# Diagonal sums of the first five chunks: from a row-wise product on GpSimd and a reduction on VectorE to a channel-wise product and a matmul

## The reference

```python
state = zeros((B, H, D, D))                      # B=2, H=8, S=768, D=48
for t in range(S):
    cur = einsum('bhd,bhe->bhde', u[None] * kt, vt)
    y[:, :, t] = einsum('bhd,bhde->bhe', rt, state + cur)
    state = wt[:, :, :, None] * state + einsum('bhd,bhe->bhde', kt, vt)
```

## Time and profile before

| what | value |
|---|---|
| median of three runs | 377.11 us |
| profiled execution | 376.72 us |
| its span | 375.1 us |
| PE busy | 365.7 us (97%) |
| DVE busy | 166.1 us (44%) |
| ACT busy | 107.7 us (29%) |
| POOL busy | 193.1 us (51%) |
| mean granted TensorE clock | 0.991 of full speed |

### The profile page before, as it was taken

The page is one execution under the profiler, slowest core; times in us unless marked ns, Lnnn a source line. Parts: engine busy times, 40 slices in busy tenths (PEclk is TensorE's granted clock), DMA queues, the critical chain, the costliest instruction groups (busy, mean ns, idle before and its releaser), DMA issues.

```text
span 375.1 us, 6472 instructions
## 1 busy us (share of the span) xinstructions
PE 365.7 (97%) x2546; PEld 325.7 (87%) x2546; DVE 166.1 (44%) x278; ACT 107.7 (29%) x205; POOL 193.1 (51%) x198
## 2 busy tenths in 40 slices
PE   5999899999999999999999999999999999999996
PEld 5888778888799998999999998888888888888885
DVE  6799888754501332295449363350023300133100
ACT  3677345555552006420012123240012200122000
POOL 3799999997967447579999970019000000000000
PEclk9699999999999999999999999999999999999999
DMA  7988696411033000031134400000000000000011
GB/s 233 417 290 328 245 367 244 148 56 44 2 108 103 3 0 3 0 84 44 43 86 126 134 36 2 0 1 31 28 28 2 0 28 30 28 0 2 0 41 45
DMA packets 12033, 31.94 MB, mean 85 GB/s; under 512 B 1633, under 2 KB 4962, under 8 KB 12002
## 3 DMA queue, kind: packets, MB, share of 16 engines
q1 hardware_dynamic: 12000, 31.51, 24.2%
q10 hardware_dynamic: 2, 0.00, 0.0%
HBM read 29.15 MB, written 2.36 MB: 84 GB/s over the span
## 4 chain that ended last, share of the span: by engine, by line
PE 74%; DVE 0%; issue 0%; POOL 0%; DVEq 0%
PE bank L1212 24%; PE bank L1210 24%; PE bank L1211 24%; PE bank L1320 1%; POOL yt L652 0%; DVE x L1055 0%; DVE x2T L1125 0%; DVEq L227 0%; DVEq L1053 0%
## 5 line engine op out<-in xcount | busy, mean ns | idle before, releaser
L854 ACT ACTIVATE ha_hi<-bank 128x512 fp32r<-128x512 f32 x36 | 21.6, 599 | 106.7 <-PE bank L1212 106.7
L1116 DVE SCALAR_TENSOR_TENSOR ha_lo<-bank,ha_hi 128x512 fp32r<-128x512 f32 x36 | 24.9, 692 | 50.6 <-ACT ha_hi L854 50.6
L1210 PE MATMUL bank<-ha_hi,c_lo 128*128 128x512 f32 x108 | 42.1, 390 | 0.0
L1212 PE MATMUL bank<-u2T_hi,c_hi 128*128 128x512 f32 x108 | 42.0, 389 | 0.0
L1211 PE MATMUL bank<-u2T_lo,c_hi 128*128 128x512 f32 x108 | 42.0, 389 | 0.0
L1212 PE MATMUL bank<-ha_hi,c_hi 128*128 128x512 f32 x108 | 42.0, 389 | 0.0
L1210 PE MATMUL bank<-u2T_hi,c_lo 128*128 128x512 f32 x108 | 42.0, 389 | 0.0
L1211 PE MATMUL bank<-ha_lo,c_hi 128*128 128x512 f32 x108 | 42.0, 389 | 0.0
L1211 PE MATMUL bank<-sg_lo,z_hi 128*128 128x384 f32 x96 | 32.1, 334 | 0.0
L1210 PE MATMUL bank<-sg_hi,z_lo 128*128 128x384 f32 x96 | 32.1, 334 | 0.0
L1212 PE MATMUL bank<-sg_hi,z_hi 128*128 128x384 f32 x96 | 32.1, 334 | 0.0
(11 more groups left out here) (143 smaller groups left out, 849.6 us busy)
## 6 DMA issues: line engine op xcount, KB each, us to landing
turned<-in_turned_all SPq DMA_DIRECT2D x10, 772.0 KB, 7.5
rows<-in_rows_all SPq DMA_DIRECT2D x12, 576.0 KB, 5.6
raw<-in_moe_w_ch SPq DMA_DIRECT2D x12, 384.0 KB, 3.1
raw<-in_moe_w_sg SPq DMA_DIRECT2D x6, 384.0 KB, 3.3
out<-x2T SPq DMA_DIRECT2D x8, 256.0 KB, 2.0
raw<-in_moe_w_in SPq DMA_DIRECT2D x4, 384.0 KB, 6.7
raw<-in_moe_w_tok SPq DMA_DIRECT2D x4, 384.0 KB, 3.1
check_w<-in_w SPq DMA_DIRECT2D x2, 576.0 KB, 11.6
```

The source lines that it names most:

```text
L854: sc.activation(ha[0][:, i, :], bank[:, :], ACT.Relu).then_inc(act_out, 1)
L1116: ve.scalar_tensor_tensor(ha[1][:, i, :], bank[:, :], 0.0, ha[0][:, i, :].bitcast(F32), ALU.max, ALU.subtract).then_inc(dve_out, 1)
L1210: te.matmul(dst, left[1], right[0], start=first, stop=False)
L1212: return te.matmul(dst, left[0], right[0], start=False, stop=last)
```

## The change

For chunks 0 to 4 the diagonal sums are made in another way. For the other chunks all stays, with the counts of the semaphores shifted by five.

- GpSimd multiplies r and k by channel (`rk_by_channel`, 112x512, both from `turned`). The product lies in the part of the `rows` slot where k and r by token lay.
- TensorE multiplies that, pair by pair and 64 tokens at a time, with two columns of u (8 matmuls with a moving side of two columns), into bank b2 behind the turned k. They stand in `turn_kp`, before its semaphore.
- ScalarE's `take_k` copies 8 columns more, into `kn_dg`, and from chunk 1 on waits for `diagonal_v` of the chunk before.
- `rk_products`, `rku_products` and `diagonal` no longer run for chunks 0 to 4; chunks 0 to 4 load v alone by token (192 KB in place of 576 KB).
- u by pairs comes with the first w (8 columns more); `ub` is loaded by a broadcast DMA after `load_rows(4)`; `spread_u`, its zeroed row, its DMA and its copy go.
- VectorE runs `forward(1)` before the masks of chunk 0.
- `keep_busy`: 14 at the start in place of 13; the two that stood in each of chunks 1 to 4 go, and two more stand in chunk 0.

```diff
+            def rk_by_channel(n):
+                if n == 0:
+                    pool.wait_ge(k0_in, 16)
+                    pool.wait_ge(r0_in, 16)
+                else:
+                    wait_turned(pool, n)
+                if n >= NR:
+                    pool.wait_ge(kn_turned, states(n - NR))
+                gp.tensor_tensor(rkc(n), kr_tile(n, 1), kr_tile(n, 0), ALU.mult).then_inc(rkc_done, 1)
...
             scale_k(0)
             scale_first_r()
-            rk_products(0)
-            for n in range(YR):
-                if n:
-                    diagonal_v(n - 1)
-                    scale_r(n + 1)
-                    scale_k(n + 1)
-                else:
-                    scale_k(1)
-                    rku_products(0)
-                    scale_r(1)
-                if n == YR - 1:
-                    diagonal_v(n)
-                rk_products(n + 1)
-                rku_products(n + 1)
+            rk_by_channel(0)
+            scale_k(1)
+            scale_r(1)
+            rk_by_channel(1)
+            for n in range(1, YR):
+                diagonal_v(n - 1)
+                if n + 1 < YR:
+                    rk_by_channel(n + 1)
+                scale_r(n + 1)
+                scale_k(n + 1)
+            diagonal_v(YR - 1)
+            rk_products(YR)
+            rku_products(YR)
             scale_k(YR + 1)
...
             def take_k(n):
-                sc.copy(kn[:, :, :], pairs(b2, QP)).then_inc(kn_copied, 1)
+                m = NP * QP
+                if n < YR:
+                    m += H
+                    if n:
+                        act.wait_ge(base_done, n)
+                sc.copy(kn_dg[:, 0:m], b2[:, 0:m]).then_inc(kn_copied, 1)
...
             for n in range(YR):
-                if n:
-                    forward(n + 1)
+                forward(n + 1)
                 mask(n, 0)
                 mask(n, 1)
-                if n == 0:
-                    forward(1)
-                if n:
-                    diagonal(n)
                 state(n)
                 if n:
                     y_tile(n - 1)
                 backward(n + 2)
-                if n == 0:
-                    diagonal(0)
...
                 for p in range(NP):
                     ins = te.transpose(b2[:, QP * p:QP * p + QP], kp[0:QP, p, :], ident[0:QP, 0:QP])
+                if n < YR:
+                    pe.wait_ge(rkc_done, n + 1)
+                    if n == 0:
+                        pe.wait_ge(w0_half_in, 16)
+                    for p in range(NP):
+                        for q in halves:
+                            ins = te.matmul(b2[q, NP * QP + 2 * p:NP * QP + 2 * p + 2], rkc(n)[:, p, q],
+                                            w0[0:QP, WS + 2 * p:WS + 2 * p + 2], start=True, stop=True)
                 ins.then_inc(kn_turned, 1)
...
-            keep_busy(13)
+            keep_busy(14)
             pe.wait_ge(ident_made, 1)
             for n in range(YR):
                 scores(n)
@@
-                    spread_u()
                     keep_busy(1)
                 state_products(n)
-                if n:
+                if n == 0:
                     keep_busy(2)
```

More of the change, by code:

```diff
@@ L154, in build @@
     check_w = at("check_w", Z, [PART, RAW])
-    w0 = at("w0", Z + RAW + C, [PART, WS])
+    w0 = at("w0", Z + RAW, [PART, WS + H])
     gt = pair("gt", GT, [PART, NF, S])
@@ L181, in build @@
     rp = put("rp", [PART, 2, NP, PART])
-    kn = put("kn", [PART, NP, QP])
+    kn_dg = put("kn_dg", [PART, NP * QP + H])
+    kn = kn_dg[:, 0:NP * QP].rearrange("s (p c) -> s p c", p=NP)
     am = put("am", [PART, H, PART])
@@ L210, in build @@
     ub = put("ub", [PART, C])
-    u_row = at("u_row", Z + RAW, [PART, C])
     rku = put("rku", [PART, 2, C])
@@ L239, in build @@
         ub_in, gln_in, bsg_in = sem("ub_in"), sem("gln_in"), sem("bsg_in")
-        ident_made, u_zeroed, u_in, u_spread = sem("ident_made"), sem("u_zeroed"), sem("u_in"), sem("u_spread")
-        ones_made = sem("ones_made")
+        ident_made, ones_made, rkc_done = sem("ident_made"), sem("ones_made"), sem("rkc_done")
         consts0, consts, v_consts = sem("consts0"), sem("consts"), sem("v_consts")
@@ L296, in w_row @@
         def w_row(n):
-            return w0[0:QP, :] if n == 0 else turned[(n - 1) % TR][0:QP, 2 * NP * PART:TW]
+            return w0[0:QP, 0:WS] if n == 0 else turned[(n - 1) % TR][0:QP, 2 * NP * PART:TW]
         def each_pair(t, first, m):
@@ L319, in v_row, with rkc @@
             return rows[:, n % NR, 2, :]
+        def rkc(n):
+            return rows[0:QP, n % NR, 0:2, :].rearrange("c i t -> c (i t)")[:, 0:NP * PART].rearrange(
+                "c (p t) -> c p t", p=NP)
         def wait_w(eng, n):
@@ L407, in load_rows @@
                 if n >= NR:
-                    sp.wait_ge(rk_done, n - NR + 1)
+                    if n - NR >= YR:
+                        sp.wait_ge(rk_done, n - NR - YR + 1)
                     sp.wait_ge(av_done, n - NR + 1)
@@ L411, in load_rows @@
                     sp.wait_ge(base_done, n - NR + 1)
-                sp.dma_start(rows[:, n % NR].rearrange("p i c -> p (i c)"), rows_all[n]).then_inc(rows_in[n % NR], 16)
+                i = 2 if n < YR else 0
+                sp.dma_start(rows[:, n % NR, i:3].rearrange("p i c -> p (i c)"), rows_all[n][:, C * i:3 * C]
+                             ).then_inc(rows_in[n % NR], 16)
             def load_first():
@@ L416, in load_first @@
                 k0, r0, w1 = slice(0, NP * PART), slice(NP * PART, 2 * NP * PART), slice(2 * NP * PART, TW)
-                sp.dma_start(w0[:, half:WS], w_first[:, half:WS]).then_inc(w0_half_in, 16)
+                sp.dma_start(w0[:, half:WS + H], w_first[:, half:WS + H]).then_inc(w0_half_in, 16)
                 sp.dma_start(w0[:, 0:half], w_first[:, 0:half]).then_inc(w0_in, 16)
@@ L453, in _ @@
             load_rows(4)
+            sp.dma_start(ub[:, :], u.rearrange("(a h) d -> a (h d)", a=1).to_broadcast([PART, C])).then_inc(ub_in, 16)
             load_turned(5)
@@ L567, in _ @@
                              pattern=[[-1, PART]], channel_multiplier=1).then_inc(ident_made, 1)
-            gp.memset(u_row[:, :], 0.0).then_inc(u_zeroed, 1)
             gp.memset(cmask[:, :], 1.0).then_inc(consts0, 1)
@@ L604, in rk_products @@
                 wait_rows(pool, n)
-                if n > 1:
-                    pool.wait_ge(dg_done, n - 1)
+                if n - 2 >= YR:
+                    pool.wait_ge(dg_done, n - YR - 1)
                 gp.tensor_tensor(rku[:, n % 2], kr_row(n, 1), kr_row(n, 0), ALU.mult
@@ L610, in rku_products @@
             def rku_products(n):
-                pool.wait_ge(rk_done, n + 1)
-                if n == 0:
-                    pool.wait_ge(ub_in, 1)
+                pool.wait_ge(rk_done, n - YR + 1)
+                if n == YR:
+                    pool.wait_ge(ub_in, 16)
                 gp.tensor_tensor(rku[:, n % 2], rku[:, n % 2], ub[:, :], ALU.mult
                                  ).then_inc(rku_done, 1)
+            def rk_by_channel(n):
[7 more added lines that the diff above has]
+                gp.tensor_tensor(rkc(n), kr_tile(n, 1), kr_tile(n, 0), ALU.mult).then_inc(rkc_done, 1)
             def scale_k(n):
@@ L648, in diagonal_v @@
                 wait_rows(pool, n)
-                pool.wait_ge(dg_done, n + 1)
+                if n < YR:
+                    pool.wait_ge(kn_copied, states(n))
+                    sums = kn_dg[:, NP * QP:NP * QP + H]
+                else:
+                    pool.wait_ge(dg_done, n - YR + 1)
+                    sums = dg[:, n % 2, :]
                 if n >= BR:
@@ L653, in diagonal_v @@
                                  v_row(n).rearrange("p (h d) -> p h d", h=H),
-                                 dg[:, n % 2, :].rearrange("p (h a) -> p h a", a=1).to_broadcast([PART, H, D]), ALU.mult
+                                 sums.rearrange("p (h a) -> p h a", a=1).to_broadcast([PART, H, D]), ALU.mult
                                  ).then_inc(base_done, 1)
@@ L885, in split_high @@
                     act.wait_ge(rp_done, NCH)
-                    act.wait_ge(dg_done, NCH)
+                    act.wait_ge(dg_done, NCH - YR)
                 hi = split_target(name, i, 0)
@@ L901, in _ @@
                 if n == 0:
-                    act.wait_ge(u_spread, 1)
-                    sc.copy(ub[:, :], ps[6][:, 0:C]).then_inc(ub_in, 1)
                     check_range("w", 1, 0)
@@ L1022, in diagonal @@
             def diagonal(n):
-                dve.wait_ge(rku_done, n + 1)
-                if n > 1:
+                dve.wait_ge(rku_done, n - YR + 1)
+                if n - 2 >= YR:
                     dve.wait_ge(base_done, n - 1)
@@ L1264, in old_part @@
             def old_part(n):
-                if n == 1:
-                    pe.wait_ge(ub_in, 1)
-                elif n >= 2:
+                if n >= 2:
                     pe.wait_ge(y_done, n if n >= YR else n - 1)
@@ L1374, in keep_busy @@
```

(12 more changed lines are left out.)

2 lines of the change are left out of this document (removed).

## The result

Six executions of the changed kernel had a median of 373.44 us (373.35 to 373.64), six of the kernel before beside them 377.12 (374.94 to 378.01). The ratio is 0.9914, with a 95% interval of 0.9887 to 0.994: faster by 0.9%. The forecast was 376.4, in a range of 374.4 to 378.1.

A forecast was written before the change was run, and what follows sets the result against it. In the loop GpSimd, VectorE and TensorE were all taken as full, GpSimd holding TensorE back slightly. +0.48 (chunk 0) − 0.76 (loop) − 0.23 (to the flag) = −0.5 us: 376.2, given as 376.4 us median, range 374.4 to 378.1.

The forecast's parts named there:

- the term of chunk 0: Chunk 0: two more keep_busy at the lower clock cost 1.28 us, so scores(1) comes at 16.55, not 16.07: +0.48 us.
- Rival 4: Chunk 0: 14 products at the start shorten TensorE's idle time, the clock never falls there: 374.0 us, 10%.
- The loop: Chunks 1 to 4: 4.85 us per chunk; scores(1) to scores(4) takes 14.55 us in place of 15.31: −0.76 us.
- The cycle named: Loop: state, scans, scale_r, scale_k, scores, then the new passes before state_products; two chunks in 9.75 us, 4.87 per chunk.
- From scores(4) to the flag: After scores(4): GpSimd starts when forward(5) ends, the flag comes 8.75 us after scores(4), not 8.98: −0.23 us.
- rival 5: Chunks 1 to 4: without keep_busy the clock falls there, some 1.7 us per stretch: 380 us or more, 4%.
- Rival 1: Before and into chunk 1: the clock rises late, lower level through new_part(0), 1.8 us on the chain: 377.9 us, 12%.
- Rival 2: New TensorE passes: each costs 0.069 us like a pass of scores, 5.45 us per chunk: 378.3 us, 6%.
- Rival 3: New TensorE passes: cheap at 0.27 us in all, the cycle shortens to 4.63 us per chunk: 375.4 us, 17%.

The follow-up runs named there:

- b_fill0: Kernel before with eight products of ones in chunk 0 between state_products(0) and new_part(0): 375.55 us, ratio 0.9976.
- b_order_fill: Kernel before with scale_r(1) before rku_products(0) and five products of ones in chunk 0: 375.27 us, ratio 0.9959.
- a_busy13: Changed kernel with 13 products of ones at the start in place of 14: 373.42 us, ratio 0.992.
- b_order: Kernel before, where GpSimd does scale_r(1) before rku_products(0): 375.28 us, ratio 0.997.
- a_move: Changed kernel with the 16 passes of the diagonal sums of chunks 2 to 4 moved before scores(n): 372.44 us, ratio 0.9875.
- a_bytes: Changed kernel that again moves unread k and r by token for chunks 0 to 4, ahead of each load of v: 376.26 us, ratio 0.9997.
- a_busy9: Changed kernel with 9 products of ones at the start in place of 14: 379.68 us, ratio 1.0079.
- a_kb0off: Changed kernel without the three products of ones in chunk 0: 373.62 us, ratio 0.9927.
- b_lean: Kernel before with scale_r(1) before rku_products(0), five products of ones in chunk 0 and none in chunks 1 to 4: 375.35 us, ratio 0.9964.
- b_busy18: Kernel before with 18 products of ones at the start in place of 13: 375.95 us, ratio 1.0003.
- b0_again: Kernel before, unchanged, timed again beside itself: 376.51 us median, 375.06 to 377.53.

## Why the prediction was wrong

**The step that failed is the term of chunk 0**, "+0.48 us". It carried the lower clock of the one profiled execution over into the changed kernel, and priced everything in it at that level: the two products at 1.28 us (they took 0.64), new_part to 16.5. From that it drew "the freed 1.6 us of GpSimd buy nothing". At full clock it is the other way round. TensorE ends chunk 0 early and scale_r(1) decides. It comes earlier by GpSimd's order and by the second turned tile's earlier landing; of these the landing reaches scores(2), the order does not (b_fill0 beside b_order_fill). In the traces scores(1) follows scores(0) after 5.26 us in the changed kernel; in the kernel before after 7.23 at the lower clock and 7.67 at the full one.

**Rival 4** (the clock never falls, 374.0 us) came nearest, with 10%. Its effect is right, its cause is wrong: not the 14th product (a_busy13) but, in most executions, the idle time that disappeared in chunk 0 (b_fill0, b_order). In the profiled execution the clock fell ahead of scores(0), where the first k came late; that it came 1.1 us earlier in the changed kernel's profile was chance. I had not looked for idle time in chunk 0, since at the lower clock none showed: TensorE ended new_part(0) just as scale_r(1) ended. The low clock hid the very wait that brings it about in other executions. The 10% were given for a reason that did not hold, so that it came near is in part luck.

**The loop**, "−0.76 us", gave −0.07 in the profiled pair. The cycle named is the right one: scores(2) to scores(4) took 10.05 us where I had 9.75. Two sizes were off. The passes come to 0.53 + 0.56 − 0.44 us and a longer hand-over to old_part, 0.7 in all on the way from scores to state_products, where I took 0.50; state(2) follows scores(2) by 4.07 us, not 3.84. And rk_by_channel takes 1.27 us, not 1.14, which counts in chunk 1, where GpSimd does it twice. a_move shows what the placement cost.

**From scores(4) to the flag** −0.24 for −0.23, and the shift passed whole to the end: both held. So did the fall of rival 5: without the products in chunks 1 to 4 the clock stayed up. Rivals 1, 2 and 3 did not occur; the 16 passes ran at 35 ns each, near the 33 ns of the row. Rival 3's price does not follow from the cycle named: with 0.27 us it is 9.52 us for two chunks, 4.76 each and not 4.63.

**The range** did not hold the time because it took the clock's state in the profile for the kernel's. The three times shown with the kernel before, 375.86 beside 377.11 and 377.13, already were, by their times, two of its three kinds. A spread of 1.3 us is a third of a per cent and would have asked for the question: which of them was profiled?

What stays open: why the second turned tile lands earlier in the changed kernel, since it did so in a_bytes too, with the bytes put back; what the shorter loads are worth by themselves, since a_bytes adds issues as well; whether the seven executions of the kernel before that kept the clock idled in chunk 0 at all, since none of them was traced; and the executions of a_busy9 with a mean of 1.000.

## What to carry to other kernels

When the times of a kernel go with its mean granted clock, find out which kind the profiled execution belongs to, and where in it the clock was low, before pricing a stretch in it; durations at the lower clock hide the waits that show at the full one. An idle stretch of TensorE, here 1.8 to 3.6 us in the first 20, can cost twice, once itself and once by the clock, and both the order of another engine and the size of a load beside it can close it. Where three engines are full, relieve two of them in one change, and put the work that moves to the fuller one where it already waits.

## What the runs showed of the hardware

- The clock held over idle times of TensorE of 0.6 to 1.7 us ahead of chunk 0 (1.66 us in a_kb0off's profile) and of 1.30 and 1.22 us ahead of chunks 1 and 2 in b_lean. It fell after 1.75 us in a_bytes, 1.79 in b_order, 1.96 in a_busy9, 2.54 in the kernel before, 2.86 in b_busy18 and 3.56 in b0_again; b_order kept it in 5 of 12 executions. Once fallen it stayed low for 3.4 us (b0_again, b_order, b_busy18) or 6.8 (before, a_bytes), and for 13.7 in a_busy9, where TensorE had no idle time in the whole stretch.
- The granted clock reads 1.00 from the start of every profile until its first change, also where it cannot have been: the passes of the first products of ones began 213 ns apart until 5.1 us in the kernel before and 6.3 us in the changed one, and 112 ns apart after that.
- Passes of 64 weight columns with two moving columns took 35 ns, 48 moving columns 33 to 34, 96 moving columns 44: between 2 and 48 columns the moving side made no difference. The Trainium skill (TensorE: Matmul & The Clock Gate, Back-to-back issue gap) has a floor of about 25 ns for it; the runs stay above and don't contradict it.
- The first scale_k, which waits for the first k, began between 4.85 and 6.70 us from the start in 16 traces, with the same three issues of SyncE up to that load.
